# Attention scores: k's low part against q's high part alone, in two 64-row tiles; 13 weight pieces instead of 14; other due times

## The reference

```python
# q, k, v: 4 batches x 8 heads x 576 positions x 64; moe: x 2304 x 512, 4 experts, 1024 hidden
scores = scale * q @ k.T
thresh = max(scores) - tau
scores = where(scores >= thresh, scores, -1e9)
attn = exp(scores - max(scores)); attn /= sum(attn) + 1e-9
x = (attn @ v) laid out as 2304 tokens x 512
p = domain_probs / (sum(domain_probs) + 1e-9)
out = sum over e of p[:, e] * (maximum(x @ w1[e], 0) @ w2[e])
```

## Time and profile before

| | |
|---|---|
| median of 3 runs | 1097.27 us (1097.25 to 1097.64) |
| the profiled execution | 1096.14 us |
| its span in the trace | 1094.4 us |
| TensorE busy | 1063.5 us (97%) |
| VectorE / ScalarE / GpSimd busy | 630.8 / 587.4 / 661.6 us |

### The profile page before, as it was taken

One profiled execution on the slowest core, in us unless ns is written; L12 is line 12 of the kernel. 1 busy time (PEld: TensorE's weight loads), 2 busy tenths in 40 slices (PEclk: granted clock), 3 DMA queues, 4 the chain that ended last, 5 costly groups with the idle time before them and its releaser, 6 DMA issues.

```text
span 1094.4 us, 17024 instructions
## 1 busy us (share of the span) xinstructions
PE 1063.5 (97%) x5752; PEld 932.3 (85%) x5752; DVE 630.8 (58%) x1216; ACT 587.4 (54%) x1137; POOL 661.6 (60%) x804
## 2 busy tenths in 40 slices
PE   5799999999999999999999999999999999999998
PEld 4798898999888888888898999998888888888887
DVE  5877686767758777777666767762122133343331
ACT  6786576757766647567465667554233242241330
POOL 6776677777886949668387878765454352222220
PEclk9999999999999999999999999999999999999999
DMA  5543343444543423323343434224242244233311
GB/s 152 147 127 98 104 137 117 121 135 142 160 138 108 131 82 105 112 70 121 98 135 104 116 112 136 77 89 133 85 127 87 68 112 148 87 106 96 106 58 38
DMA packets 96788, 121.08 MB, mean 111 GB/s; under 512 B 41152, under 2 KB 45248, under 8 KB 96704
## 3 DMA queue, kind: packets, MB, share of 16 engines
q1 hardware_dynamic: 96400, 119.68, 37.0%
q10 hardware_dynamic: 304, 0.33, 0.1%
HBM read 115.25 MB, written 4.72 MB: 110 GB/s over the span
## 4 chain that ended last, share of the span: by engine, by line
PE 83%; POOL 6%; DVE 4%; ACT 2%; issue 2%; DMA 2%; SPq 1%; ACTq 0%; DVEq 0%
PE e_ps L860 12%; PE e_ps L862 12%; PE e_ps L861 12%; PE e_ps L847 10%; PE e_ps L845 10%; PE e_ps L846 10%; PE t_ps L791 5%; PE s_ps L779 3%; PE x_ps L818 3%; PE s_ps L780 3%; POOL w_lo L757 3%; PE x_ps L820 2%; DVE q_hl L973 1%; DMA stage<-w 1%; POOL p L745 1%
## 5 line engine op out<-in xcount | busy, mean ns | idle before, releaser
L757 POOL TENSOR_TENSOR w_lo<-stage,w_hi 128x512 fp32r<-128x512 f32 x272 | 356.0, 1317 | 244.1 <-ACT w_hi L951 241.0
L951 ACT ACTIVATE w_hi<-stage 128x512 fp32r<-128x512 f32 x320 | 194.0, 625 | 174.3 <-PE e_ps L862 115.4
L845 PE MATMUL e_ps<-x_hi,w_hi 128*128 128x512 f32 (+1 forms) x640 | 240.5, 376 | 0.0
L847 PE MATMUL e_ps<-x_hi,w_lo 128*128 128x512 f32 (+1 forms) x640 | 236.4, 369 | 0.0
L846 PE MATMUL e_ps<-x_lo,w_hi 128*128 128x512 f32 (+1 forms) x640 | 236.1, 369 | 0.0
L860 PE MATMUL e_ps<-w_hi,h_hi 128*128 128x512 f32 x576 | 229.8, 399 | 0.0
L862 PE MATMUL e_ps<-w_hi,h_lo 128*128 128x512 f32 x576 | 225.0, 391 | 0.0
L861 PE MATMUL e_ps<-w_lo,h_hi 128*128 128x512 f32 x576 | 224.7, 390 | 0.0
L1032 DVE SCALAR_TENSOR_TENSOR h_lo<-e_ps,h_hi 128x512 fp32r<-128x512 f32 (+1 forms) x160 | 101.9, 637 | 136.1 <-ACT h_hi L941 135.0
L941 ACT ACTIVATE h_hi<-e_ps 128x512 fp32r<-128x512 f32 (+1 forms) x160 | 88.3, 552 | 107.3 <-PE e_ps L847 106.9
L847 PEld LDWEIGHTS e_ps<-x_hi,w_lo 128*128 128x128 f32 x640 | 120.5, 188 | 15.4
(11 more groups left out here) (63 smaller groups left out, 1482.8 us busy)
## 6 DMA issues: line engine op xcount, KB each, us to landing
stage<-w SPq DMA_DIRECT2D x320, 256.0 KB, 2.9
k_raw<-kT SPq DMA_DIRECT2D x94, 144.0 KB, 2.8
v_raw<-v SPq DMA_DIRECT2D x40, 128.0 KB, 2.2
out<-acc SPq DMA_DIRECT2D x18, 256.0 KB, 2.0
q_raw<-qT SPq DMA_DIRECT2D x32, 144.0 KB, 3.0
q_raw<-qT SPq DMA_DIRECT2D x16, 96.0 KB, 2.6
v_raw<-v SPq DMA_DIRECT2D x80, 16.0 KB, 2.2
q_raw<-qT SPq DMA_DIRECT2D x16, 80.0 KB, 2.3
```

Source lines behind the costliest of these rows:

```text
L757: gp.tensor_tensor(w_lo[:, m % RING, :], stage[:, m % STAGES, :], w_hi[:, m % RING, :], ALU.subtract).then_inc(s_wl, 1)
L845: mm(ps[:, 0:n], w_hi[:, piece, tile], x_hi[:, k, cols], start=k == 0, stop=False)
L847: op = mm(ps[:, 0:n], w_lo[:, piece, tile], x_hi[:, k, cols], start=False, stop=k == KT - 1)
L951: run(w_hi[:, m % RING, :], stage[:, m % STAGES, :], copy).then_inc(s_wh, 1)
```

## The change

For the scores, low part of k times low part of q is left out: k's low part meets q's high part alone. That product has 64 rows for each half of the keys, so the two halves are given to two tiles of the array, rows 0 to 63 for the first 288 keys and rows 64 to 127 for the others, each with its own PSUM bank. A unit first runs its two (or four) 128-row matmuls against `k_hh` and then its two (or four) 64-row matmuls against `k_ll`.

For this q's high part is needed in all 128 rows: a new tile `q_hh` holds it in the 64 rows in which `q_hl` holds the low part. ACT writes both with two 64-row operations in place of one with 128 rows, and `q_lo` is counted from `q_hh`. Which 64 rows of `q_hl` hold the low part now alternates with the turn. The new tile needs 2.5 KB per partition; `RING` goes from 14 to 13, which frees 4 KB. Two small memsets on GpSimd clear the edges of `q_hh`. The tables of due times are new, and `takes()` counts `q_hi` as two operations.

```diff
-RING = 14
+RING = 13
...
-PLAN = dict(first=-1.79, period=2.89, experts=16.98, end=13.3, weights=31.7, weight=8.16, prob=21.1)
+PLAN = dict(first=0.47, period=2.99, experts=15.19, end=13.93, weights=31.34, weight=8.33, prob=22.52)
...
-    if name in ("q_hi", "q_lo"):
+    if name == "q_hi":
+        return 2 * (PAIRS[x // 2].n * 0.00095 + 0.2)
+    if name == "q_lo":
         return PAIRS[x // 2].n * 0.00095 + 0.25
...
+        q_hh = sb("q_hh", [P, PAD], F32R)
...
+            gp.memset(q_hh[:, SEQ:PAD].bitcast(F32), 0.0).then_inc(s_zero, 1)
+            gp.memset(q_hh[:, 0:PAD - SEQ].bitcast(F32), 0.0).then_inc(s_zero, 1)
...
                         for turn, c0 in uses:
-                            tile, last = q_hl[turn % 2][:, c0:c0 + P], (turn, c0) == uses[-1]
-                            mm(ps[:, c, :], tile, k_hh[turn % 2][:, cols], start=(turn, c0) == uses[0], stop=False)
-                            op = mm(ps[:, c, :], tile, k_ll[turn % 2][:, cols], start=False, stop=last)
+                            mm(ps[:, c, :], q_hl[turn % 2][:, c0:c0 + P], k_hh[turn % 2][:, cols],
+                               start=(turn, c0) == uses[0], stop=False)
+
+                    for turn, c0 in uses:
+                        for c in range(2):
+                            tile = (q_hl[turn % 2] if c == turn % 2 else q_hh)[c * HD:(c + 1) * HD, c0:c0 + P]
+                            keys = k_ll[turn % 2][c * HD:(c + 1) * HD, c * HALF:(c + 1) * HALF]
+                            op = mm(ps[:, c, :], tile, keys, start=False, stop=(turn, c0) == uses[-1],
+                                    tile_position=(c * HD, 0))
...
-                    run(q_hl[turn % 2][:, q_cols(turn)], q_raw[:, 0:n], copy, scale=tau_col[:, 3:4]).then_inc(s_qhi, 1)
+                    for tile, rows in ((q_hl[turn % 2], main_rows(turn)), (q_hh, other_rows(turn))):
+                        op = run(tile[rows, q_cols(turn)], q_raw[rows, 0:n], copy, scale=tau_col[rows, 3:4])
+                    op.then_inc(s_qhi, 1)
...
-                    lo = q_hl[turn % 2][HD:P, q_cols(turn)]
-                    ve.scalar_tensor_tensor(out=lo, in0=q_raw[HD:P, 0:n], scalar=tau_col[HD:P, 3:4],
-                                            in1=lo.bitcast(F32), op0=ALU.mult, op1=ALU.subtract).then_inc(s_qlo, 1)
+                    rows = other_rows(turn)
+                    lo, hi = (tile[rows, q_cols(turn)] for tile in (q_hl[turn % 2], q_hh))
+                    ve.scalar_tensor_tensor(out=lo, in0=q_raw[rows, 0:n], scalar=tau_col[rows, 3:4],
+                                            in1=hi.bitcast(F32), op0=ALU.mult, op1=ALU.subtract).then_inc(s_qlo, 1)
```

More of the change, by code:

```diff
@@ L206, in ups_through @@
     return (UPS_TO[t - 1] if t else 0) + (f + 1) * len(col_parts(CHUNKS[t // E][0]))
[L212 to L217, removed]
-PLAN = dict(first=-1.79, period=2.89, experts=16.98, end=13.3, weights=31.7, weight=8.16, prob=21.1)
+ALONE = dict(load=-8.34, q_hi=7.54, q_lo=16.44, k_hi=0.15, k_lo=-10.72, v_hi=13.98, v_lo=0.21, max=5.61, thr=12.84,
+             exp=4.03, mask=1.7, eps=12.12, rec=-4.16, norm=13.55, tr=-4.48, phi=1.6, plo=8.84, pv=14.31, xo=22.87,
+             xs=19.59, x_hi=7.08, x_lo=12.11)
+AMONG = dict(load=-9.84, q_hi=2.37, q_lo=-2.55, k_hi=0.87, k_lo=-6.94, v_hi=-4.34, v_lo=9.42, max=-1.23, thr=2.62,
+             exp=8.85, mask=3.35, eps=6.79, rec=6.88, norm=-3.19, tr=10.29, phi=6.88, plo=8.44, pv=14.77, xo=5.3,
+             xs=11.77, x_hi=12.07, x_lo=8.32)
+PLAN = dict(first=0.47, period=2.99, experts=15.19, end=13.93, weights=31.34, weight=8.33, prob=22.52)
 def halves_of(u):
@@ L647, in build @@
         block = ctx.enter_context(nc.Block())
-        ZEROS = 6
+        ZEROS = 8
         TURNS32 = 2 * SOLID_PAIRS
```

## The result

The changed kernel takes **1131.72 us** (median of 4 runs, 1129.97 to 1133.58), the kernel before 1097.45 us beside it. The ratio is 1.0315, 95% interval 1.0299 to 1.0330: 34 us slower. The profiled execution took 1132.26 us with a span of 1130.5 us, 36.1 us more than the span before.

A forecast was written before the change was run, and what follows sets the result against it. TensorE's matmul stream was taken to bound the kernel from 116 us on, a waiting pipeline up to 85 us. Terms −11.7 + 2.0 + 1.0 = −8.7 us gave 1088.6 us; range for 8 in 10: 1079 to 1122.

The forecast's parts named there:

- Part 1: Score matmuls among the experts, the main term: 64-row pairs replace 128-row ones and save 89 ns a use, −11.7 us.
- The first of its two bounds: Score matmuls among the experts: tiles fully side by side, loads done ahead, a pair costs 133 ns; 17.6 us less.
- The middle between the two bounds: Score pairs among the experts: 89 ns a use, between 17.6 us less (loads ahead) and 5.8 (loads one after another).
- Rival 1: Score matmuls: changing between 128 and 64 rows stops the array, twice a unit; 1108 to 1146 us, chance 0.32.
- Part 2: First 85 us: ACT's `q_hi` becomes two operations, the second counted at full price; +2.0 us.
- The first item: At the start, `q_lo` waits for both `q_hi` operations before the first scores; +0.6 us.
- Part 3: ACT among the experts: second `q_hi` operations mostly covered by idle time; +1.0 us, between 0 and 4.
- Part 4: 13 weight places: high parts may start one piece later, but slack covers it; 0 us, at most 6.
- Part 5: The new order: TensorE has little idle time after 116 us to win or lose; 0, with 2 us either side.
- Rivals 2 and 3: 2: tiles do not overlap, 1098 to 1100 us, chance 0.14. 3: late weights, 1094 us, within the forecast's 0.54.

The follow-up runs named there:

- e4: The changed kernel with every pair of 64-row matmuls issued twice in a row, so the low part is added twice: 1149.45 us, ratio 1.0476.
- e1: The changed kernel with k's low part through 128-row matmuls again; its order, 13 weight places and doubled q step stay: 1107.04 us, ratio to before 1.0087.
- e11: e1 with the two 64-row tiles in the 27 units ahead of the experts alone: 1108.96 us, ratio 1.0105.
- e7: The kernel before with q's high part written by two 64-row ACT operations, both into `q_hl`, nothing else: 1105.85 us, ratio 1.0074.
- e9: The kernel before with e5's order word for word, but 14 weight places: 1107.57 us, ratio 1.0087.
- e5: The kernel before with `RING = 13`, its order settled anew for that number: 1106.88 us, ratio 1.0089.
- e6: The kernel before with the changed kernel's tables of due times, 14 places and one q step: 1106.47 us, ratio 1.0085.
- e2: The changed kernel with the kernel before's tables of due times; tiles, 13 places and doubled q step stay: 1138.13 us, ratio 1.0371.
- e8: e1 with the kernel before's tables: no tiles, 13 places, two q steps, new `takes()`: 1117.59 us, ratio 1.0172.
- e3: The changed kernel with each half of the keys doing its 128-row then its 64-row matmuls, four row-count changes a unit: 1203.29 us, ratio 1.0966.
- e10: The changed kernel without the second tile, so the second half of the keys lacks its low product: 1130.49 us, ratio 1.0301.

## Why the prediction was wrong, point by point

**Part 1, the step that failed.** The forecast stood on the assumption that the change of row count has no price. It has one, 0.20 us. The first of its two bounds was exactly right for the overlap: the tiles start 3 ns apart, their loads run side by side, and the pair costs 0.13 us (e4). So there was a gain of 132 × 0.133 = 17.6 us, and 2 × 0.20 us in each of 117 units, 47 us, stood against it: +29 us instead of −11.7. Run against run the tiles cost 24.7 us (e1); the difference is in part given back by shorter waits and in part open (e11). The middle between the two bounds had no ground either: loads are not done one after the other.

**Rival 1 was the case that came true**, with 0.32. It gave 1108 for exposed loads alone and 1146 with the whole modelled tail of 0.16 us; the load is 0.11 us as read from the earlier trace rows, the emptying 0.09 and not 0.16. With these the rival's own sum is 117 × (2 × 0.20 − 0.133) − 2.0 = 29.2 us, plus 3.0: 1129.5. That this is 2 us from the measured 1131.7 is partly luck, since the tiles cost 24.7 and not 29.2 us in the total, and the rest 9.6 and not 3.0. The range ended at 1122 since half of the rival was put below it; between its two mechanisms nothing in the trace decided, and the range should have reached on. The argument against it, that transposes come and go without a price, was a wrong analogy: they have 128 rows as well.

By the Trainium skill (TensorEngine Tiling, Key Properties) a change of the tiling mode drains TensorE. The trace agrees, with 0.09 us between the last column and the next load, at each of the two borders, and none between pairs of the same mode (e4). I cited this and then gave the forecast to the other case.

**Part 2** foresaw +2.0 us for the first 85 us, and the first expert matmul came 1.1 us later, in e7 2.6 us. e7 is the clean test, and 2.6 is near 2.0, but not for the reasons given. The first item did not show: I expected the first scores at 9.0 us and they came at 8.19 (8.09 in e7), see the last section.

**Part 3** was priced at 1.0 us by one occurrence on the chain; e7 puts it at 8.0 − 2.6 = 5.4 us. ACT's busy time on the page is up by 35.7 us and not by 29, but the price of the operations was right: they take 768 and 776 ns for 576 columns against 766 before, and the durations of all ACT operations add up to 29.8 us more. The page counts a moment once where two records overlap, and they overlap less now. The step that failed was to count as hidden what is not on the chain now. Idle time of 36% does not tell how much slack a given step has.

**Part 4** said that a place less does not make weights late, and it does not; e9 prices the place itself at nothing in that order. It overlooked that the same constant goes into `settle()` and gives another order, which costs 9 us (e5, e9).

**Part 5** was given 0 ± 2 us because TensorE's idle time is small. That bounds what an order can win, not what it can lose. e6 shows +9 us. Each set of tables is the better one in its own kernel: the new ones lose 9 us in the kernel before, and win 6.4 (e2) and 10.6 us (e8) with the changed kernel's parts.

**Rivals 2 and 3** did not come true: the tiles overlap, and no expert matmul waits for `w_lo`.

So 34.3 us are 24.7 for the tiles (the changed kernel less e1) and 9.6 for the rest (e1 less before). The rest is not a sum of its parts: alone, they cost 9, 9 and 8 us.

## What to carry to other kernels

Count the borders before you pack matmuls into row tiles. Here each change between 128 and 64 rows cost 0.20 us and each pair saved 0.13 us of 288 columns. By these numbers (an estimate, no such kernel was run) a visit needs more than three such pairs before it gains; one pair a visit does not pay. Other column counts and tiles of 32 rows were not run. And where an order has been fitted to a kernel, price any edit that touches it by what it can lose: three edits that were each "hidden" or "neutral" by the busy times cost 8 to 9 us apiece. A constant that also feeds the planner is two edits; try the order and the resource apart, as e9 does.

## What the runs showed of the hardware that I had not expected

**The load after a change starts only 0.09 us after the last column**, although loads within one row count run a whole matmul ahead (e3, e4). It does so in both directions, and for a single 64-row matmul too (e10).

**DVE's `q_lo` takes half the time in some places.** The first one, 64 rows of 384 columns, took 1.29 us before and 0.66 us in the changed kernel:

```profile
6.12 1.40 POOL L732 TENSOR_TENSOR k_ll<-k_raw,k_hh 128x576 fp32r<-128x576 f32 x1 [3.09 <-ACT k_hh L903]
...
7.27 0.66 DVE L988 SCALAR_TENSOR_TENSOR q_hl<-q_raw,small,q_hh 64x384 fp32r<-64x384 f32 x1 [3.10 <-ACT q_hh L896]
```

Before, GpSimd's `k_ll` ran from 6.35 to 7.75 us and `q_lo` from 6.88, so most of `q_lo` lay beside it; here it started 0.25 us before GpSimd was through. It is not a matter of the other operand tile alone: in e7, which keeps the old operands, the first `q_lo` took 0.67 us too. So the doubled step ended 0.39 us later but `q_lo` was 0.62 us shorter; with k's arrival, after which `k_hi` began at 5.35 and not 5.58 us, this is why the first scores were not late.

Nothing was run on it, but nearly all `q_lo` of the traces fit one rule: a `q_lo` that starts while a GpSimd operation is under way ends when that operation is through, plus its free time (0.62 us for 384 columns, 0.82 for 576), less 0.20 us. For the first one before, that is 7.75 + 0.62 − 0.20 = 8.17; it ended at 8.16. In the traces of before, after and e7, 95 `q_lo` start with over 0.22 us of a GpSimd operation left, and 93 of them end within 0.03 us of this. Another of the changed kernel, where 1.42 + 0.82 − 0.20 gives 2.04 us from 645.16:

```profile
645.16 1.42 POOL L732 TENSOR_TENSOR k_ll<-k_raw,k_hh 128x576 fp32r<-128x576 f32 x1
645.20 2.00 DVE L988 SCALAR_TENSOR_TENSOR q_hl<-q_raw,small,q_hh 64x576 fp32r<-64x576 f32 x1 [1.47 <-ACT q_hh L896]
```

Of 27 with less than that left, 23 took their free time and 4 over 1 us more. All 22 that start while GpSimd stands still take their free time. `q_lo`'s length thus depends on what GpSimd has begun before it, and an order changes that.

**After a wait of 2.9 us the clock was low.** In the changed kernel TensorE stands from 569.5 us until a transpose's input is normalised. Afterwards its matmuls of 384 columns start 0.32 us apart, and not 0.17, until 579.65 us, and the granted clock of that stretch is 0.50: 1.2 and not 2.4 GHz. Timeline of PE, and a row of the busy times by stretch, with the clock behind POOL's:

```profile
569.52 0.28 PE L830 MATMUL x_ps<-pt_hi,v_hl 128*128 128x256 f32 x1
572.47 0.85 PE L803 MATMUL t_ps<-ident,p 128*128 128x128 f32 x5 [2.67 <-POOL p L751]
573.37 0.85 PE L784 MATMUL s_ps<-k_hh,q_hl 128*128 128x288 f32 x2
...
575.00:577.00 2.00, 2.00 (x7) 2.00 (x7) 1.14 (x4) 0.92 (x2) 1.83 (x4) 0.50 0.25 74
```

14 recorded distances of this kind cost some 2 us more. e8 shows the same after a wait of 3.8 us that ends at 564.6 us. The kernel before has no such stretch after 91 us, but it has one from 88 to 91 us (granted clock 0.50), which costs 1.4 us and which the changed kernel lacks; so little of the 36 us comes from the clock.
